# Own term of the first four attention units on TensorE, with more dummies and the gate product moved

## Chip, core and metric

One core of one Trainium2 chip runs the whole kernel. The metric is device time in microseconds (us). Engines are called as in the profile: PE (TensorE, with PEld for its weight loads), DVE (VectorE), ACT (ScalarE), POOL (GpSimd) and SP (SyncE, which issues most of the DMAs).

## What is computed

Three stages follow each other: a linear attention with decays, a dense MLP with a squared ReLU, and a mixture of 8 experts that picks one expert for each token. Only the first has a part in the change:

```python
def _attn_ref(r, k, v, w, u):          # B, H, S, D = 4, 8, 768, 48
    for t in range(S):
        cur = np.einsum('bhd,bhe->bhde', u[None] * kt, vt)
        y[:, :, t] = np.einsum('bhd,bhde->bhe', rt, state + cur)
        state = wt[:, :, :, None] * state + np.einsum('bhd,bhe->bhde', kt, vt)
```

The term `cur` is the token's own term: for head h and token t it adds v[t] times the number sum over d of r[t,d] u[d] k[t,d]. The kernel computes this number for each token and head, and puts it on the diagonal of the matrix of scores. The MLP is `h = max(x @ w_in, 0); (h * h) @ w_out`, and the gate of the experts is a product with the MLP's output.

## The kernel before

**Tiling.** The 768 tokens fall into C = 6 chunks of T = 128. A *unit* (c, b) is chunk c of batch b, with all 8 heads as PAIRS = 4 pairs; 24 units in all. Features lie on partitions: the first head of a pair on partitions 0 to 47, the second on 64 to 111, and the 16 between are padded. `rk_in` holds r and k in this layout, `w_dec` the decays. The MLP of chunk i runs on PE while the attention of chunk i + 1 goes on at its side. So only the four units of chunk 0 stand alone, ahead of everything; the change touches these.

**One unit.** `decays` (DVE, L1193, a scan) makes running products `cum` of the decays; `inverse` (DVE, L1207, two halves) their reciprocals. On POOL `receptance` (L1604) multiplies r by `cum`, `keys` (L1625) k by the reciprocals. On PE `head_scores` (L654) makes the scores. `own_rows` (POOL, L1614 and L1616) multiplies r, k and u from a second copy of r and k with tokens on partitions (`own`, 384 KB a unit, loaded by `load_own`, L406); `own_term` (DVE, L1227) sums over each head's 48 features into `own_sum`; `own_diagonal` (ACT, L978) writes eight diagonal matrices into `scores`. `mask_scores` (DVE, L1215, two instructions) lays the scores above the diagonal over them; it waits for `ps_scores` and `sb_diag`. Then PE goes on with `k_transpose` (L663), `attention` (L683 to L693) and `growth` (L729). ACT takes `k_nat` (L956) and `xt_hi` (L965, `take_xhi`), DVE `xt_lo` (L1259, `take_xlo`). The last `take_xlo` of chunk 0 releases `layer1` of the MLP (L602 to L604).

**Order.** Each engine has its own program, in an order written by hand, and they meet only in semaphores. For chunk 0 this order stands at L832 to L843 (PE), L1085 to L1100 (ACT), L1453 to L1480 (DVE) and L1699 to L1708 (POOL); SP's list of loads begins at L461. `keep_busy(n)` (L830) issues n dummy products of 128x512 on PE, which nobody reads: six ahead of unit 0, two behind the scores of units 1 and 2. `gate_product(0)` (L740) is an unrelated product for the gate, of `gate_w` with 768 KB of transposed `w_out` (`load_transposed(0)`, L425); it stands behind unit 2's growth. `split_hi` (ACT, L944) and `split_lo` (DVE, L1418, or POOL, L1653) split the MLP's weights (`load_mlp_piece`, L420, 768 KB each) into two parts. `early_decays`, `early_rk` and `early_v` are loads for unit n that wait until unit n - 2 is done with the buffer. SP issues in order, so that a load behind a waiting one waits too.

**Buffers.** `own` lies in `spare`, for the odd units of chunk 0 in `stage[1]`. HID[0] and HID[1] are the two PSUM banks of layer 1, unused ahead of it but for the dummies (HID[1]).

Of the kernel before, what the change touches and what calls it, by code (L numbers as in the profile page):

```python
# [18 lines left out]
ALU = mybir.AluOpType  # L19
# [7 lines left out]
T = 128  # L27
# [6 lines left out]
def build(nc, rkw, rk_rows, v, u_rows, w_in, w_out, w_out_t, w_gate, w1, w2, out):  # L34
# [29 lines left out]
    with ExitStack() as ctx:  # L64
        def sb(name, shape, dt=F32):
            return ctx.enter_context(nc.sbuf_tensor(name, shape, dt))
# [57 lines left out]
        k_nat = sb("k_nat", [T, PAIRS, PK])  # L124

# [79 lines left out]
        u_loaded = sem("u_loaded")  # L205
        pad_set = sem("pad_set")
# [164 lines left out]
        def _(sp):  # L371
# [26 lines left out]
            def load_own(c, b):  # L398

                unit = B * c + b  # L400
                if isinstance(c, int) and 2 <= unit <= B:
                    sp.wait_ge(own_summed, unit - 1)
                elif not isinstance(c, int) or unit > 2:
                    sp.wait_ge(own_summed, unit)
                unit = unit % UNITS
                sp.dma_start(own_of(c, b), rk_rows[bass.ds(unit, 1)].rearrange("x t d -> (x t) d")  # L406
                             ).then_inc(own_loaded[b % 2], 16)
# [56 lines left out]
            load_own(0, 0)  # L464
            sp.dma_start(own_u[:, :], u_rows).then_inc(u_loaded, 16)
            load_rk(0, 0, 1)
            sp.wait_ge(const_v, 2)
            load_rk(0, 0, 0)
            load_decays(0, 1, 1)
# [4 lines left out]
            load_own(0, 1)  # L474
# [4 lines left out]
            load_own(0, 2)  # L479
# [4 lines left out]
            load_own(0, 3)  # L484
            load_transposed(0)
            early_rk(3)
            early_v(3)
            early_decays(4)
            load_own(1, 0)
            load_mlp_piece(1)  # L490
# [108 lines left out]
        def _(pe):  # L599
# [232 lines left out]
            keep_busy(6)  # L832
            for b in range(B):
                head_scores(0, b)
                if b == 1 or b == 2:
                    keep_busy(2)
                k_transpose(0, b)
                attention(0, b)
                growth(0, b)
                if b == 2:  # L840
                    pe.wait_ge(const_dma, 16)
                    gate_product(0)
# [97 lines left out]
        def _(act):  # L940
# [40 lines left out]

            def side(n, c, cg, par, c_last, per=8):
# [102 lines left out]
            keep_decay(0)  # L1085
            own_diagonal(0, 0)
            keep_decay(1)
            for b in range(B):
                if b == 1:
                    split_hi(0)  # L1090
                if b == 1 or b == 2:
                    keep_decay(b + 1)
                if b == 3:
                    take_gate(0)
                    split_hi(1)
                take_k(0, b)
                if b < B - 1:
                    own_diagonal(0, b + 1)
                take_xhi(0, 0, b)
# [81 lines left out]
        def _(dve):  # L1181
# [38 lines left out]
            def own_term(c, b):  # L1220

                unit = B * c + b
                n = b % 2
                dve.wait_ge(own_done, 2 * unit + 2)
                if not isinstance(c, int) or unit > 1:
                    dve.wait_ge(sb_diag, unit - 1)
                dve.tensor_reduce(own_sum[:, n, :], own_of(c, b)[:, 0:DM].rearrange("p (h d) -> p h d", h=H), AX.X,  # L1227
                                  ALU.add).then_inc(own_summed, 1)
# [209 lines left out]
            dve.memset(x_cur[:, 0:KD * GW], 0.0)  # L1438
            dve.memset(rk_in[0][32:64].rearrange("p a j t -> p (a j t)"), 1.0).then_inc(const_v, 1)
# [15 lines left out]
            own_term(0, 0)  # L1455
# [5 lines left out]
            own_term(0, 1)  # L1461
            for b in range(2):
                decays(0, b + 2)
                inverses(0, b + 2)
                mask_scores(0, b + 1, 0)
                mask_scores(0, b + 1, 1)
                own_term(0, b + 2)
                take_xlo(0, 0, b)
# [4 lines left out]
            own_term(1, 0)  # L1473
            take_xlo(0, 0, 2)
            take_xlo(0, 0, 3)
            inverse(1, 0, 0)
# [114 lines left out]
        def _(pool):  # L1591
# [14 lines left out]
            def own_rows(c, b):  # L1606

                unit = B * c + b
                n = b % 2
                pool.wait_ge(own_loaded[n], (2 * c + b // 2) * 16 + 16)  # L1610
                if isinstance(c, int) and unit == 0:
                    pool.wait_ge(u_loaded, 16)
                rows = own_of(c, b)
                pool.tensor_tensor(rows[:, 0:DM], rows[:, 0:DM], rows[:, DM:2 * DM], ALU.mult).then_inc(own_done, 1)  # L1614
                pool.wait_ge(own_done, 2 * unit + 1)
                pool.tensor_tensor(rows[:, 0:DM], rows[:, 0:DM], own_u[:, :], ALU.mult).then_inc(own_done, 1)  # L1616

# [10 lines left out]
            def factors(c, b, own_first=False):  # L1628

                if own_first:  # L1630
                    own_rows(c, b)
                    receptance(c, b)
                else:
                    receptance(c, b)
                    own_rows(c, b)
                keys(c, b)
# [62 lines left out]
            for b in range(2):  # L1699
                factors(0, b, own_first=True)  # L1700
            own_rows(0, 2)
            receptance(0, 2)
            keys(0, 2)
            factors(0, 3, own_first=True)
# [112 lines left out]
```

## Time and profile before

| | |
|---|---|
| median of 3 runs | 778.81 us (777.79 to 779.17) |
| the profiled execution | 779.41 us |
| its span | 777.8 us |
| busy: PE, DVE, ACT, POOL | 755.1, 469.6, 323.7, 229.3 us |
| granted clock over the span | 0.991 |
| first product of layer 1 starts at | 40.75 us |

The four units of chunk 0, from the timelines (start of the instruction, us):

| unit | scores (PE) | diagonal (ACT) | mask (DVE) | transposes (PE) | PE idle ahead of them |
|---|---|---|---|---|---|
| (0,0) | 12.48 | 9.76 | 13.82 | 15.21 | 1.56 |
| (0,1) | 18.26 | 17.50 | 22.61 | 23.95 | 2.02 |
| (0,2) | 25.98 | 25.68 | 29.47 | 30.81 | 1.75 |
| (0,3) | 33.64 | 32.55 | 35.20 | 36.58 | 1.78 |

How to read it: a row of a timeline has the start and the length of an instruction, engine, line, operation and tiles (written <- read); brackets show how long the engine had been idle and who released it. Line numbers are those of the kernel before. The chain of waits is followed back from the last instruction, at each step to what released it. PEclk is the granted share of TensorE's full clock: 1.00 is 2.4 GHz, 0.50 is 1.2 GHz.

### The profile page before, as it was taken

The page shows a single profiled execution, that of the slowest core. Times are in us where ns is not written, and L with a number is a line of the kernel's source. Part 1 is how long each engine was busy: PE and PEld are TensorE (multiplying, and loading weights), DVE is VectorE, ACT ScalarE, POOL GpSimd, SP SyncE. Part 2 cuts the span into 40 slices and gives each one's busy share as a digit, 9 for nine tenths or more (in the row PEclk, how much of TensorE's full clock was granted, in tenths as well). Part 3 has the DMA queues.
Part 4 walks back from the last instruction along what each step waited for, and adds up shares of the span by engine and source line. Part 5 has one row for each costly group of instructions (what it writes and reads, how often), then busy time and mean ns, then how long its engine had stood idle before and what let it go on. Part 6 is the DMA issues. An engine that isn't in the chain of part 4 may idle for free.

```text
span 777.8 us, 15695 instructions
## 1 busy us (share of the span) xinstructions
PE 755.1 (97%) x5571; PEld 661.1 (85%) x5571; DVE 469.6 (60%) x756; ACT 323.7 (42%) x636; POOL 229.3 (29%) x213
## 2 busy tenths in 40 slices
PE   6799999999999999999999999999999999999994
PEld 3488888888988888888888899998999999999994
DVE  8977887866586576676486645334542246353861
ACT  3555544434333334434344323253432255253841
POOL 7834423312242222421042210262431112211211
PEclk9999999999999999999999999999999999999998
DMA  9875222321132223322331005154661126616610
GB/s 231 270 227 186 69 67 86 109 62 41 44 111 63 62 63 102 93 62 62 101 95 40 23 33 203 58 190 138 227 233 61 61 62 214 224 55 224 212 52 7
DMA packets 50195, 87.99 MB, mean 113 GB/s; under 512 B 5932, under 2 KB 33560, under 8 KB 50128
## 3 DMA queue, kind: packets, MB, share of 16 engines
q1 hardware_dynamic: 41376, 61.01, 27.5%
q0 software_dynamic: 7648, 24.51, 8.7%
q10 hardware_dynamic: 1104, 1.57, 0.6%
q8 instruction: 43, 0.70, 0.4%
q14 instruction: 24, 0.20, 0.1%
HBM read 72.78 MB, written 16.75 MB: 115 GB/s over the span
## 4 chain that ended last, share of the span: by engine, by line
PE 91%; DVE 3%; ACT 1%; issue 1%; POOL 1%; DMA 1%; SPq 0%; DVEq 0%; POOLq 0%; ACTq 0%
PE bank L602 27%; PE bank L604 25%; PE bank L603 25%; PE bank L654 3%; PE bank L874 3%; PE bank L683 2%; PE bank L699 2%; PE bank L729 1%; PE bank L663 1%; PE bank L821 1%; ACT spare L978 1%; DVE spare L1215 1%; DVE work L1193 1%; PE bank L688 1%; PE bank L693 1%
## 5 line engine op out<-in xcount | busy, mean ns | idle before, releaser
L602 PE MATMUL bank<-wo_hi,h_hi 128*128 128x394 f32 (+1 forms) x576 | 201.6, 350 | 1.0 <-DVE h_lo L1505 1.0
L604 PE MATMUL bank<-wo_hi,h_lo 128*128 128x394 f32 (+1 forms) x576 | 196.1, 340 | 0.0
L603 PE MATMUL bank<-wo_lo,h_hi 128*128 128x394 f32 (+1 forms) x576 | 195.6, 340 | 0.0
L1383 DVE SCALAR_TENSOR_TENSOR hid<-bank,hid 128x512 f32<-128x512 f32 x96 | 65.2, 679 | 135.0 <-ACT hid L1020 135.0
L1020 ACT ACTIVATE hid<-bank 128x512 f32<-128x512 f32 x96 | 57.0, 594 | 158.3 <-PE bank L604 149.9
L602 PE MATMUL bank<-xt_hi,wi_hi 128*128 128x512 f32 x288 | 116.5, 405 | 0.3 <-DVE xt_lo L1259 0.3
L602 PEld LDWEIGHTS bank<-wo_hi,h_hi 128*128 128x128 f32 x576 | 108.3, 188 | 9.0 <-issue 3.0
L604 PE MATMUL bank<-xt_hi,wi_lo 128*128 128x512 f32 x288 | 113.0, 392 | 0.0
L603 PE MATMUL bank<-xt_lo,wi_hi 128*128 128x512 f32 x288 | 112.7, 391 | 0.0
L603 PEld LDWEIGHTS bank<-wo_lo,h_hi 128*128 128x128 f32 x576 | 108.5, 188 | 2.9
L1604 POOL TENSOR_TENSOR work<-work 112x512 f32<-112x512 f32 x24 | 35.6, 1484 | 251.6 <-DVE work L1193 249.7
L604 PEld LDWEIGHTS bank<-wo_hi,h_lo 128*128 128x128 f32 x576 | 108.4, 188 | 0.0
L1029 ACT ACTIVATE h_hi<-hid 128x512 fp32r<-128x512 f32 x96 | 60.6, 631 | 86.3 <-DVE hid L1383 85.2
L1744 POOL DMA_INDIRECT out<-odds,y_idx x26 | 26.9, 1033 | 172.4 <-DVE odds L1517 153.7
L1389 DVE TENSOR_TENSOR h_lo<-hid,h_hi 128x512 fp32r<-128x512 f32 x96 | 66.5, 693 | 17.6 <-ACT h_hi L1029 17.2
L1207 DVE RECIPROCAL odds<-work 112x256 f32<-112x256 f32 x44 | 76.6, 1745 | 0.7
L978 ACT ACTIVATE spare<-ident,own_sum 128x128 f32<-128x128 f32 x192 | 58.7, 388 | 33.4 <-DVE own_sum L1227 27.1
L1111 ACT ACTIVATE hid<-bank 128x512 f32<-128x512 f32 x48 | 28.7, 597 | 87.7 <-PE bank L604 81.7
L604 PEld LDWEIGHTS bank<-xt_hi,wi_lo 128*128 128x128 f32 x288 | 54.0, 188 | 12.3
L602 PEld LDWEIGHTS bank<-xt_hi,wi_hi 128*128 128x128 f32 x288 | 54.0, 188 | 11.9 <-issue 2.0
L1322 DVE TENSOR_TENSOR xt_lo<-bank,xt_hi 128x384 fp32r<-128x384 f32 x25 | 13.9, 557 | 81.8 <-ACT xt_hi L1038 81.8
L603 PEld LDWEIGHTS bank<-xt_lo,wi_hi 128*128 128x128 f32 x288 | 54.1, 188 | 8.3
(152 smaller groups left out, 1221.3 us busy)
## 6 DMA issues: line engine op xcount, KB each, us to landing
work<-rkw SPq DMA_DIRECT2D x48, 192.0 KB, 3.8
spare<-rk_rows SPq DMA_DIRECT2D x22, 384.0 KB, 4.2
work<-sorted_rows SPq DMA_DIRECT2D x24, 193.0 KB
work<-rkw SPq DMA_DIRECT2D x48, 96.0 KB, 3.3
work<-v_rows SPq DMA_DIRECT2D x24, 192.0 KB, 3.9
x_cur<-sorted_rows SPq DMA_DIRECT2D x24, 192.0 KB
work<-w POOLq DMA_DIRECT2D x6, 768.0 KB, 7.4
x<-w POOLq DMA_DIRECT2D x6, 768.0 KB, 10.1
```

The source lines that it names most:

```text
L602: pe.matmul(ps, a_hi, b_hi, start=start, stop=False, skip_group_check=True)
L603: pe.matmul(ps, a_hi, b_lo, start=False, stop=False, skip_group_check=True)
L604: return pe.matmul(ps, a_lo, b_hi, start=False, stop=stop, skip_group_check=True)
L978: last = act.activation(scores[:, h % 2, h // 2, :], ident[:, :], ACT.Copy, scale=own_sum[:, b % 2, h:h + 1])
L1020: act.activation(hid[:, f % 2, :], HID[f % 2][:, :], ACT.Relu).then_inc(sb_relu, 1)
L1029: act.activation(h_hi[:, f % 3, :], hid[:, f % 2, :], ACT.Copy).then_inc(sb_hhi, 1)
L1111: act.activation(hid[:, half, :], banks[2 + half][:, :], ACT.Relu).then_inc(e_relu, 1)
L1207: dve.reciprocal(inv_of(c, b)[0:PK, :].rearrange("p (j t) -> p j t", j=PAIRS)[:, two], by_time(cum[b % 2])[0:PK, two, 1:T + 1]).then_inc(i ...
L1383: dve.scalar_tensor_tensor(hid[:, f % 2, :], HID[f % 2][:, :], 0.0, hid[:, f % 2, :], ALU.max, ALU.mult).then_inc(sb_sq, 1)
L1389: dve.tensor_tensor(h_lo[:, f % 3, :], hid[:, f % 2, :], h_hi[:, f % 3, :].bitcast(F32), ALU.subtract).then_inc(sb_hlo, 1)
L1604: pool.tensor_tensor(r, r, by_time(cum[n])[0:PK, :, 0:T], ALU.mult).then_inc(r_done, 1)
L1744: pool.indirect_dma_start(out=out, out_offset=bass.IndirectOffsetOnAxis(ap=y_idx[:, n:n + 1], axis=0), in_=y_out[:, n, :], in_offset=None, ...
```

## The change

The own term of units (0,0) to (0,3) is made in another way; from unit (1,0) on it is as before.

- POOL: `first_own(b)` multiplies r by k in the layout with features on partitions, ahead of `receptance`, one instruction of 112x512 in place of the two of `own_rows`. It needs the unit's `rk` load only.
- PE: `own_products(b)` multiplies this product (as the stationary side, 112x128 a pair) by `u_two`, four products with two columns, which sums over the features and weights by u. It writes 8 columns of HID[0]. For unit 0 it stands between three and two dummies, for units 1 to 3 behind the attention of the unit before and ahead of its growth.
- ACT: `take_own(b)` copies 128x8 from PSUM to `own_sum`, ahead of the diagonal. DVE's `own_term` is gone for these units, and that of (1,0) stands behind the last two `take_xlo`.
- SP: the loads of `own` for these units are gone; `u_two` comes in two small loads of single elements; `own_u` and `own (1,0)` come later; `load_mlp_piece(1)` comes earlier, `load_transposed(0)` later, behind the loads of unit 3 and ahead of `early_decays(4)`.
- Dummies: 3 + 2 ahead of unit 0 (6 before), one behind the scores of unit 0 (none), two for units 1 and 2 as before, one for unit 3 (none). `gate_product(0)` moves from behind unit 2's growth to behind unit 3's scores. ACT's `split_hi(1)` moves from unit 3 to unit 2.

```diff
@@ SP
-            load_own(0, 0)
-            sp.dma_start(own_u[:, :], u_rows).then_inc(u_loaded, 16)
             load_rk(0, 0, 1)
             sp.wait_ge(const_v, 2)
             load_rk(0, 0, 0)
+            for half in range(2):
+                p = slice(HALF * half, HALF * half + D)
+                src = u_rows[0:1, :].rearrange("x (j a d) -> a d (x j)", a=2, d=D)
+                sp.dma_start(u_two[p, :, half], src[half], allow_slow_non_contiguous=True).then_inc(u_two_loaded, 16)
...
-            load_own(0, 1)
...
-            load_own(0, 2)
             load_mlp_piece(0)
             early_decays(3)
             early_rk(2)
             early_v(2)
-            load_own(0, 3)
-            load_transposed(0)
+            load_mlp_piece(1)
             early_rk(3)
             early_v(3)
+            load_transposed(0)
             early_decays(4)
+            sp.dma_start(own_u[:, :], u_rows).then_inc(u_loaded, 16)
             load_own(1, 0)
-            load_mlp_piece(1)
@@ PE
+            def own_products(b):
+                pe.wait_ge(own_done, 2 * b + 2)
+                if b > 0:
+                    pe.wait_ge(own_summed, b)
+                rows = by_time(own_of(0, b)[:, 0:PAIRS * T])
+                for j in range(PAIRS):
+                    last = pe.matmul(HID[0][:, 2 * j:2 * j + 2], rows[0:PK, j, :], u_two[0:PK, j, :],
+                                     start=(j == 0), stop=(j == PAIRS - 1), skip_group_check=True)
+                last.then_inc(ps_own, 1)
-            keep_busy(6)
+            keep_busy(3)
+            pe.wait_ge(u_two_loaded, 32)
+            own_products(0)
+            keep_busy(2)
             for b in range(B):
                 head_scores(0, b)
-                if b == 1 or b == 2:
+                if b == 0:
+                    keep_busy(1)
+                elif b < B - 1:
                     keep_busy(2)
+                else:
+                    pe.wait_ge(const_dma, 16)
+                    gate_product(0)
+                    keep_busy(1)
                 k_transpose(0, b)
                 attention(0, b)
+                if b < B - 1:
+                    own_products(b + 1)
                 growth(0, b)
-                if b == 2:
-                    pe.wait_ge(const_dma, 16)
-                    gate_product(0)
@@ ACT
+            def take_own(b):
+                act.wait_ge(ps_own, b + 1)
+                act.activation(own_sum[:, b % 2, :], HID[0][:, 0:H], ACT.Copy).then_inc(own_summed, 1)
             keep_decay(0)
+            take_own(0)
             own_diagonal(0, 0)
...
+                if b == 2:
+                    split_hi(1)
                 if b == 3:
                     take_gate(0)
-                    split_hi(1)
                 take_k(0, b)
                 if b < B - 1:
+                    take_own(b + 1)
                     own_diagonal(0, b + 1)
                 take_xhi(0, 0, b)
@@ DVE
+            dve.memset(u_two[:, :, :], 0.0)
...
-            own_term(0, 0)
...
-            own_term(0, 1)
...
-                own_term(0, b + 2)
...
-            own_term(1, 0)
             take_xlo(0, 0, 2)
             take_xlo(0, 0, 3)
+            own_term(1, 0)
@@ POOL
+            def first_own(b):
+                pool.wait_ge(loaded[b % 2], (b // 2) * 32 + 32)
+                if b > 1:
+                    pool.wait_ge(own_summed, b - 1)
+                pool.tensor_tensor(by_time(own_of(0, b)[:, 0:PAIRS * T])[0:PK], rk_in[b % 2][0:PK, 0],
+                                   rk_in[b % 2][0:PK, 1], ALU.mult).then_inc(own_done, 2)
-            for b in range(2):
-                factors(0, b, own_first=True)
-            own_rows(0, 2)
-            receptance(0, 2)
-            keys(0, 2)
-            factors(0, 3, own_first=True)
+            for b in range(B):
+                first_own(b)
+                receptance(0, b)
+                keys(0, b)
```

## Rows read from the trace of the kernel before

**Rows 1.** Stretches of the trace: busy us of each engine (instructions), granted clock, DMA share.

```profile
40.75:777.00 736.25, 726.38 (x5254) 643.04 (x5254) 434.75 (x715) 305.22 (x587) 195.34 (x173) 1.00 0.34 105
```

**Rows 2.** The chain of waits, 0 to 50 us: start, us, what ended last.

```profile
39.52 0.50 ACT xt_hi L965
40.05 0.57 DVE xt_lo L1259
```

**Rows 3.** DVE's timeline, 4 to 36 us: start, us, engine, line, operation, tiles.

```profile
5.50 3.36 DVE L1207 RECIPROCAL odds<-work 112x256 f32<-112x256 f32 x2
...
13.82 1.34 DVE L1215 COPY_PREDICATED spare<-before,bank 128x512 f32<-128x512 int32 x2 [0.66 <-PE bank L654]
...
16.70 0.50 DVE L1227 TENSOR_REDUCE own_sum<-stage 128x8 f32<-128x384 f32 x1
17.11 2.18 DVE L1193 TENSOR_TENSOR_SCAN work<-work,odds 112x516 f32<-112x516 f32 x1
...
22.61 1.28 DVE L1215 COPY_PREDICATED spare<-before,bank 128x512 f32<-128x512 int32 x2
...
24.70 1.46 DVE L1193 TENSOR_TENSOR_SCAN work<-work,odds 112x516 f32<-112x516 f32 x1
...
29.47 1.28 DVE L1215 COPY_PREDICATED spare<-before,bank 128x512 f32<-128x512 int32 x2
...
33.54 1.73 DVE L1418 TENSOR_TENSOR wi_lo<-stage,wi_hi 128x1536 fp32r<-128x1536 f32 x1
35.20 1.33 DVE L1215 COPY_PREDICATED spare<-before,bank 128x512 f32<-128x512 int32 x2
```

**Rows 4.** ACT's timeline, 30 to 41 us, the diagonal and a small copy.

```profile
32.55 2.45 ACT L978 ACTIVATE spare<-ident,own_sum 128x128 f32<-128x128 f32 x8 [0.56 <-PE bank L683]
...
40.50 0.20 ACT L1077 ACTIVATE wo_hi<-bank 128x40 fp32r<-128x40 f32 x1 [0.49 <-PE bank L748]
```

**Rows 5.** Stretches again: the granted clock (column PEclk) behind two pauses of PE.

```profile
16.00:20.00 4.00, 3.94 (x65) 3.26 (x55) 3.96 (x4) 2.89 (x10) 3.07 (x2) 0.57 1.08 274
36.60:40.00 3.40, 3.40 (x52) 2.63 (x52) 0.82 (x2) 1.33 (x3) 3.40 (x5) 0.50 1.01 370
```

**Rows 6.** POOL's timeline: one receptance, keys (0,0), keys (0,1).

```profile
9.10 1.18 POOL L1604 TENSOR_TENSOR work<-work 112x512 f32<-112x512 f32 x1
10.23 2.20 POOL L1625 TENSOR_TENSOR work<-work,odds 112x512 f32<-112x512 f32 x1
...
16.93 1.27 POOL L1625 TENSOR_TENSOR work<-work,hid 112x512 f32<-112x512 f32 x1 [0.99 <-DVE hid L1207]
```

**Rows 7.** PE's weight loads of the dummies, 8 to 10 us.

```profile
8.55 0.34 PEld L830 LDWEIGHTS bank<-odds,before 128*128 128x128 f32 x1 [0.52 <-issue]
9.35 0.19 PEld L830 LDWEIGHTS bank<-odds,before 128*128 128x128 f32 x1 [0.46 <-issue]
```

**Rows 8.** PE's timeline, 12 to 31 us: scores, two dummies, transposes.

```profile
12.48 1.16 PE L654 MATMUL bank<-work 48*128 48x128 f32 x16 [0.40 <-POOL work L1625]
...
19.94 1.98 PE L830 MATMUL bank<-odds,before 128*128 128x512 f32 x4
...
30.81 0.60 PE L663 MATMUL bank<-ident,work 112*128 112x112 f32 x4 [1.75 <-DVE spare L1215]
```

**Rows 9.** DMA issues, 24.5 to 27.4 us: line, KB each, us to landing.

```profile
work<-rkw SPq DMA_DIRECT2D x2, 192.0 KB, 3.2
```

**Rows 10.** DMA issues, 19.0 to 19.5 us.

```profile
x<-w_out_t SPq DMA_DIRECT2D x1, 768.0 KB, 6.4
```

**Rows 11.** DMA issues, 6.4 to 7.1 us.

```profile
work<-v_rows SPq DMA_DIRECT2D x1, 192.0 KB, 7.2
x_cur<-w_gate SPq DMA_DIRECT2D x1, 15.0 KB, 7.0
```

**Rows 12.** DMA issues, 35.2 to 36.5 us.

```profile
stage<-w_out SPq DMA_DIRECT2D x1, 768.0 KB, 10.1
work<-rkw SPq DMA_DIRECT2D x2, 96.0 KB, 8.8
```

More of the change, by code:

```diff
@@ L124, in build @@
         k_nat = sb("k_nat", [T, PAIRS, PK])
+        u_two = sb("u_two", [T, PAIRS, 2])
         state = spare[:, 2 * DM + 8 * T:].rearrange("p (b j d) -> p b j d", b=B, j=PAIRS)
@@ L205, in build @@
         u_loaded = sem("u_loaded")
+        u_two_loaded = sem("u_two_loaded")
+        ps_own = sem("ps_own")
         pad_set = sem("pad_set")
@@ L400, in load_own @@
                 unit = B * c + b
[L401 to L404, printed above, removed]
+                sp.wait_ge(own_summed, B - 1 if isinstance(c, int) and unit == B else unit)
                 unit = unit % UNITS
@@ L1224, in own_term @@
                 dve.wait_ge(own_done, 2 * unit + 2)
-                if not isinstance(c, int) or unit > 1:
-                    dve.wait_ge(sb_diag, unit - 1)
+                dve.wait_ge(sb_diag, unit - 1)
                 dve.tensor_reduce(own_sum[:, n, :], own_of(c, b)[:, 0:DM].rearrange("p (h d) -> p h d", h=H), AX.X,
@@ L1609, in own_rows @@
                 n = b % 2
-                pool.wait_ge(own_loaded[n], (2 * c + b // 2) * 16 + 16)
-                if isinstance(c, int) and unit == 0:
+                pool.wait_ge(own_loaded[n], (2 * c + b // 2 - 2) * 16 + 16)
+                if isinstance(c, int) and unit == B:
                     pool.wait_ge(u_loaded, 16)
@@ L1626, in keys, with factors @@
                                    ).then_inc(k_done, 1)
[L1628 to L1635, printed above, removed]
+            def factors(c, b):
+                receptance(c, b)
+                own_rows(c, b)
                 keys(c, b)
```

## The prediction

> **What bounds the kernel now.** I read first the busy time by stretch [rows 1]. From 40.75 us on, where chunk 0 of the first layer begins, PE is busy in 726.4 of the 736.25 us that are left. Nothing of the change touches these products, so the change can pay only by letting that first layer start earlier, and what it shifts there is carried to the end one for one.
>
> Then the chain of waits of the stretch ahead [rows 2]. It enters through the load of `own_u` and POOL's own rows of unit 0, and ends with attention (0,3), `take_xhi` at 39.52 and `take_xlo` at 40.05. Between them it runs mostly through DVE, whose timeline [rows 3] the reader should lay out as a row of masks: (0,0) at 13.82, (0,1) at 22.61, (0,2) at 29.47, (0,3) at 35.20, each 1.3 us. From 13.82 to 36.5 DVE has no pause. So the units are paced by DVE, except where the diagonal on ACT is later. For unit 3 it is nearly so: ACT's diagonal runs 32.55 to 35.00 [rows 4], DVE's `split_lo(0)` 33.54 to 35.27, and the mask starts at 35.20.
>
> Last, the clock. From 36.6 to 40 PE is granted 0.50, the 1.2 GHz level [rows 5], after it had had nothing to do between the scores and the transposes of unit 3. Unit 3 takes 39.52 - 36.53 = 2.99 us from the end of its mask to the end of attention; unit 2, at 2.4 GHz, 32.55 - 30.75 = 1.80.
>
> **Part by part, first the start.** Removed from POOL: two products in each of units 0 to 3, and four loads of 384 KB. Added: one product of r and k of the shape of `receptance`, 1.18 us [rows 6]. `own_u` leaves the first queue places. The first product needs `rk(0,0)` alone, which now has two decay halves ahead of it; I put its landing at 6.1 us. The product ends at about 7.3, receptance at 8.5, and keys wait for the reciprocals, which end at 8.86 as now [rows 3]. DVE goes straight on to the scan of unit 1, and keys then share their time with it as at 10.23, where they took 2.20 us [rows 6]: 9.0 to 11.3, not 12.43.
>
> This gain of 1.1 us is not all kept, since PE's own queue is now in the way. Passes of a dummy come 0.85 us apart until 9.2 and 0.43 after that; the weight loads show the step from 0.34 to 0.19 us [rows 7]. Three dummies are six passes, 4.15 to 9.25. Then come the four own products, eight passes with two columns each. No row shows such a product. Bounds: a pass of the scores costs 1.16/16 = 0.07 us, one of the transposes, which also load wide weights, 0.60/4 = 0.15 [rows 8]; so 0.6 to 1.2 us. I take 0.85, between them. Two more dummies are 4 passes, 1.72 us by the row of four in 1.98, less the tail. Scores (0,0): 9.25 + 0.85 + 1.72 = 11.8, to 13.0; the mask starts at 13.15 after 13.82, a gain of 0.7. The diagonal is ready just before: products out at 10.2, `take_own` 0.20 like the small copy of [rows 4], diagonal 2.45, so 13.0.
>
> The Trainium skill, "TensorE: Matmul & The Clock Gate", section "LDWEIGHTS (loading the stationary operand)", has the load's time as columns/1.2, however little streams after it: it speaks against using 128 weight columns for 2 results. An estimate by it is 8 x 107 ns = 0.86 us, and the sum would come out the same.
>
> **DVE from mask to mask.** After mask (0,0), one reciprocal of 1.75 us ends at 16.1. Before, `own_term` (16.70 to 17.1) followed, and then the scan took 2.18 us because keys (0,1) had started 0.18 us ahead of it [rows 3, 6]. Now the scan comes directly, ahead of POOL, and takes 1.23: it ends at 17.4, not 19.3. Two reciprocals of 3.4: mask (0,1) at 20.75, gain 1.85. POOL's keys (0,1) end at 18.7, scores at 19.9: not late. The next scan, 24.70 now, would be due at 22.4, but rk(0,2) is issued at 15.2, lands 3.2 to 4 us after its issue where little is queued [rows 9], and then product, receptance and keys follow, 1.2 each: keys hold the port until about 23.2 and the scan ends at 24.4. Mask (0,2) at 27.7, gain 1.8.
>
> **Unit 3, where the added wait sits.** Removed: `own_term` from DVE. Added, in series: own products on PE behind attention (0,2), 0.85, then `take_own`, 0.20, and two hand-overs, 0.1. The diagonal waited for attention alone until now, and the last mask is queued behind it. From the end of mask (0,2), 29.0: attention ends at 30.7 (+1.7 as in unit 2), diagonal starts at 31.85, ends at 34.3, mask at 34.45. So 1.8 shrinks to 0.75 us. For units 1 and 2 the same wait is covered: their diagonals end at 19.8 and 27.4, ahead of masks at 20.75 and 27.7.
>
> Other waits into this mask: the scan of (1,0) needs `early_decays(4)`, now behind the 768 KB of `load_transposed(0)`, which itself moved from 19.12 to about 24.9. The queue then holds some 1.3 MB at about 300 KB/us, so the decays land at 30.6; scan 1.25 and split 1.73 [rows 3] end at 33.6, 0.8 us before they cost anything.
>
> **The clock and the gate product.** Between scores and transposes of unit 3 PE now has the gate product (0.86 us) and a dummy (0.86), and its pause shrinks to under 1 us. If it keeps 2.4 GHz, this returns 2.99 - 1.80 = 1.2 us. Cost of the gate product: it needs `transposed`, issued at 24.9; by the 6.4 us of [rows 10] it lands at 31.3 at the latest, scores (0,3) end at 32.8. It is hidden, with the two ending at 34.5, a us before the transposes can start.
>
> **Costed at nothing:** the two `u_two` loads, 384 elements of 4 B. The gate weights came as 384 pieces of 40 B and landed 0.27 us after the v rows ahead of them (6.92 + 7.0 against 6.45 + 7.2) [rows 11]; `u_two` has until 9.25. The Trainium skill, "DMA: Bandwidth & Descriptors", section "Rules for kernel authors", warns that such a load becomes one descriptor for each element; the trace's 0.27 us for as many pieces decides. `own_term(1,0)` moves behind the last `take_xlo` and delays the first `square` by 0.5 us; layer 1 has its other bank, so PE does not see it. Dummies of units 0 and 1 lie in pauses that masks end.
>
> **The sum.** Mask (0,3) 0.75 us earlier, 1.2 us of clock: 1.95, call it 2.0. The profiled execution has 779.41 us (span 777.8, 1.6 around it), 0.6 over the median of 778.81. By its own sum it becomes 777.4, and the median 776.8 us. A measurement can tell about 0.2%, 1.56 us, from no change.
>
> **Rivals.** (1) The clock is 1.2 GHz in unit 3 all the same: the pause is shorter but there, and between 16 and 20 us, behind the pause ahead of 15.2, PE also had 0.57 [rows 5]. Then 0.8 us of gain stays: 778.0. Against it: units 1 and 2 have two dummies in this place, and their transposes run at 2.4 (0.60 us, as the row of unit 2 has it [rows 8]).
> (2) The diagonal's new wait is longer (own products at their upper bound or at 1.2 GHz, up to +0.85), so that the last mask is no earlier than now: 777.6 to 778.
> (3) Slower: `early_decays(4)` behind the transposed weights. The same load issued at 35.7 behind three large pieces took 8.8 us, and the last of these pieces 10.1 [rows 12]. Issued at 25.5 the decays would land at 34.3 to 35.6, the last mask would start at 37.4 to 38.7, 2.2 to 3.5 us later than before, and the clock gives 1.2 back: 779.8 to 781.1. It costs from a landing of 31.4 on and turns the whole change into a loss from 33.4. Against it: fewer bytes are queued than at 35.7.
> (4) It does not do what it says: POOL and DVE are relieved, but scans and keys fall into each other's time otherwise than I laid out (a scan held as the one of 2.18 us), 0.9 us lost at one of three places: 777.8.
> (5) More than forecast: own products at 0.07 us a pass, keys (0,2) earlier: 776.0.
>
> **How the numbers follow.** Forecast 776.8, 0.50; (5) 0.08; (1) 0.15; (2) and (4) together 0.17; (3) 0.10. Faster by over 0.2% (under 777.25): 0.58, the forecast and (5); slower (over 780.4): 0.07, the upper part of (3); within it 0.35, the rest. Range 775.6 to 779.1: the lower end is (5) with 0.4 for the spread of the runs, the upper end takes in (1) and (4) with that spread and leaves out most of (3).
>
> **What would show it.** Masks of DVE at 13.1, 20.8, 27.7 and 34.4; an own product of about 0.85 us after each attention; diagonal (0,3) starting 1.1 us after attention (0,2) ended; a granted clock of 1.00 at the transposes of unit 3; the first product of layer 1 at 38.8. A pause of DVE ahead of the scan of (1,0) would be rival 3, a long wait of the gate product the same load seen from PE. The forecast is wrong if the stretch after 40 us isn't carried one for one.

## The result and the profile after

| | before | after |
|---|---|---|
| median, us (12 runs each) | 778.74 (777.79 to 779.25) | 783.23 (779.96 to 784.25) |
| the profiled execution, its span, us | 779.41, 777.8 | 783.07, 781.5 |
| granted clock over the span | 0.991 | 0.991 |
| first product of layer 1 at, us | 40.75 | 40.30 |

The ratio of after to before is 1.0053, interval 1.0043 to 1.0064: the change makes the kernel slower by half a per cent, where 776.8 us was forecast and 775.6 to 779.1 was the range.

The stretch that the change touches is not where it went. Layer 1 starts 0.45 us earlier than before. The lead can be followed through DVE's copies of `logits`, one mark for each chunk: 298.76 against 299.19 us in before, still 0.43 ahead, and then 388.53 against 384.00, 4.53 behind.

DVE's timeline of before and of after around 300 us, start, us, engine, line, operation, tiles, and in brackets the idle time ahead and its releaser; before is the first fence.

```profile
299.19 0.24 DVE L1395 COPY logits<-bank 128x10 f32<-128x10 f32 x2 [2.53 <-PE bank L604]
299.36 1.02 DVE L1404 COPY x<-bank 128x384 f32<-128x384 f32 x2
301.94 0.69 DVE L1383 SCALAR_TENSOR_TENSOR hid<-bank,hid 128x512 f32<-128x512 f32 x1 [1.56 <-ACT hid L1020]
302.55 1.37 DVE L1215 COPY_PREDICATED spare<-before,bank 128x512 f32<-128x512 int32 x2
...
304.40 1.23 DVE L1193 TENSOR_TENSOR_SCAN work<-work,odds 112x516 f32<-112x516 f32 x1
...
384.00 0.24 DVE L1395 COPY logits<-bank 128x10 f32<-128x10 f32 x2 [2.53 <-PE bank L604]
```

```profile
298.76 0.24 DVE L1422 COPY logits<-bank 128x10 f32<-128x10 f32 x2 [2.53 <-PE bank L604]
298.93 1.02 DVE L1431 COPY x<-bank 128x384 f32<-128x384 f32 x2
303.36 0.69 DVE L1410 SCALAR_TENSOR_TENSOR hid<-bank,hid 128x512 f32<-128x512 f32 x1 [3.41 <-issue]
306.02 1.33 DVE L1243 COPY_PREDICATED spare<-before,bank 128x512 f32<-128x512 int32 x2 [1.97 <-issue]
...
307.84 1.22 DVE L1221 TENSOR_TENSOR_SCAN work<-work,odds 112x516 f32<-112x516 f32 x1
...
388.53 0.24 DVE L1422 COPY logits<-bank 128x10 f32<-128x10 f32 x2 [2.53 <-PE bank L604]
```

In before DVE's pause at 300.4 ends with ACT's `hid`, which it needed. In after ACT's `hid` is done at 300.92 + 0.60 = 301.52, and DVE starts at 303.36, released by "issue", which is time in which it waited for nothing that the profile shows; behind this one instruction comes a second such pause. The scan is at 307.84 against 304.40: the 0.43 us of lead have become 3.44 of lag. Two things mark the place. It is where DVE's loop over two chunks at a time (L1510 of after, `dve.Fori`) jumps back to its start, for the only time (it runs twice). And the DMA view shows loads of instructions there. Its rows for 299 to 308 us (queue, kind, packets, MB, share of 16 engines), first before, then after:

```profile
q8 instruction: 1, 0.02, 0.6%
```

```profile
q14 instruction: 3, 0.02, 0.8%
```

The row of q8 doesn't belong to the jump: between 200 and 480 us a load of 16 KB on q8 comes about every 10 to 25 us in both traces, in after at 308.7, just behind the window. The three of 8 KB on q14 are what is new. By the trace they start at 301.3, 304.0 and 306.5 us, behind the jump, while before has no load on q14 between 282.7 and 313.1.

The chain of waits of after, 295 to 312 us (start, us, what ended last), runs through the pause, and PE's own rows (stretch: length, busy of PE, PEld, DVE, ACT and POOL, granted clock, DMA share, GB/s) show who pays, before first:

```profile
299.06 0.07 DVEq L1510
299.13 0.28 issue
299.41 0.55 DVE x L1431
299.95 3.27 issue
303.22 0.09 DVEq L1510
303.36 0.10 DVE hid L1410
303.46 2.35 issue
```

```profile
299.95:306.20 6.25, 6.25 (x83) 5.09 (x85) 4.66 (x7) 2.65 (x6) 0.49 (x1) 1.00 0.65 213
```

```profile
299.95:306.20 6.25, 4.21 (x29) 2.96 (x27) 0.88 (x3) 1.71 (x3) 0.00 (x0) 1.00 0.59 203
...
304.00:308.00 4.00, 0.76 (x4) 0.60 (x4) 2.03 (x5) 1.11 (x2) 0.00 (x0) 0.91 0.01 4
308.00:312.00 4.00, 4.00 (x63) 3.16 (x62) 3.96 (x4) 1.04 (x2) 2.78 (x3) 0.66 0.02 4
```

PE runs dry behind DVE (0.76 us busy of the 4 from 304 on), and as it comes back the granted clock falls: 0.66 from 308 to 312, where before had 1.00. That is where the further 1.1 us from +3.44 to +4.53 go. On PE itself the transposes of this unit come 3.00 us later than in before (the two rows below, before first), and from them to the next product of layer 1 PE takes 3.73 us (307.40 to 311.13) where before took 2.15 (304.40 to 306.55), for the same work: 3.00 + 1.58 = 4.58 behind. At the end of the span +3.7 is left.

```profile
304.40 0.55 PE L663 MATMUL bank<-ident,work 112*128 112x112 f32 x4
```

```profile
307.40 1.01 PE L663 MATMUL bank<-ident,work 112*128 112x112 f32 x4 [3.24 <-DVE spare L1243]
```

**The stretch ahead of layer 1.** Rows of after that answer to [rows 3, 4, 5, 8], from the timelines of DVE, PE and ACT and the view of stretches:

```profile
13.89 1.33 DVE L1243 COPY_PREDICATED spare<-before,bank 128x512 f32<-128x512 int32 x2 [1.96 <-PE bank L654]
...
21.26 1.30 DVE L1243 COPY_PREDICATED spare<-before,bank 128x512 f32<-128x512 int32 x2
...
29.02 1.36 DVE L1243 COPY_PREDICATED spare<-before,bank 128x512 f32<-128x512 int32 x2 [0.75 <-ACT spare L998]
33.20 1.23 DVE L1221 TENSOR_TENSOR_SCAN work<-work,odds 112x516 f32<-112x516 f32 x1 [2.38 <-DMA work<-rkw]
34.35 1.73 DVE L1445 TENSOR_TENSOR wi_lo<-stage,wi_hi 128x1536 fp32r<-128x1536 f32 x1
36.00 1.34 DVE L1243 COPY_PREDICATED spare<-before,bank 128x512 f32<-128x512 int32 x2
```

```profile
9.41 1.40 PE L840 MATMUL bank<-u_two,spare 112*128 112x2 f32 x8
...
20.15 3.40 PE L830 MATMUL bank<-odds,before 128*128 128x512 f32 x4
23.34 0.86 PE L663 MATMUL bank<-ident,work 112*128 112x112 f32 x4
```

```profile
33.28 2.45 ACT L998 ACTIVATE spare<-ident,own_sum 128x128 f32<-128x128 f32 x8
```

```profile
22.00:24.00 2.00, 2.00 (x6) 0.78 (x4) 2.00 (x3) 0.41 (x2) 1.78 (x2) 0.50 0.89 334
36.60:40.00 3.40, 2.37 (x53) 1.79 (x53) 1.57 (x4) 1.24 (x3) 3.32 (x4) 1.00 1.03 379
```

The clock came back in unit 3 as forecast (1.00 where [rows 5] have 0.50). But it fell in unit 1: the same four passes of dummies that took 1.98 us in [rows 8] took 3.40, and the transposes behind them came 0.78 us after the mask's end (22.56). Unit 2's mask then waited 0.75 us for its diagonal. And the scan of unit (1,0) waited 2.38 us for its decays; through it and the split the last mask was at 36.00, 0.80 later than in before.

### The profile page after: what moved, and what is told of

Read it like the earlier page. It is cut to its first block, busy times and chain, and to the rows that moved or that the text cites. A ratio compares the mean times of both kernels' runs of the same rounds, so it can differ in the third digit from the quotient of the medians.

```text
span 781.5 us, 15764 instructions
## 1 busy us (share of the span) xinstructions
PE 760.3 (97%) x5605; PEld 664.9 (85%) x5605; DVE 467.6 (60%) x753; ACT 324.5 (42%) x640; POOL 223.0 (29%) x209
## 4 chain that ended last, share of the span: by engine, by line
PE 92%; DVE 3%; issue 2%; DMA 1%; ACT 1%; SPq 0%; DVEq 0%; POOL 0%; POOLq 0%; ACTq 0%
PE bank L602 27%; PE bank L604 25%; PE bank L603 25%; PE bank L654 3%; PE bank L894 3%; PE bank L699 2%; PE bank L683 2%; PE bank L830 1%; PE bank L729 1%; PE bank L663 1%; PE bank L821 1%; DMA work<-rkw 1%; PE bank L688 1%; PE bank L693 1%; DVE spare L1243 1%
```

## Experiments

Theory A: DVE's loss at 300 us is a wait for its own instructions at the loop's jump back, and whether there is one hangs on where the loop lies in DVE's program. Ahead of the jump's branch DVE's trace has 531 instructions of all kinds in before and 526 in after (four `own_term` and two waits less, one memset more). Theory B: it is a consequence of the change's work or timing, such as later loads, the clock, or POOL and DVE meeting otherwise.

**The five instructions put back, as ones that do nothing** (one column each of a tile that nobody reads).

```diff
@@ DVE, before the first decays
+            for n in range(5):
+                dve.memset(unused[:, n:n + 1], 0.0)
```

> The changed kernel, with five one-column memsets of a tile that nobody reads, on DVE ahead of mask (0,0), where DVE waits anyway. The change takes five instructions (four own terms and two waits gone, one memset new) from DVE's program ahead of its loop over chunks; in its trace DVE stands still for 3.41 and 1.97 us at 300 us, where the loop's first pass ends, with three 8 KB instruction loads beside it. Theory (the loop's place in DVE's program decides whether its code has to be loaded again at the jump): the pauses at 300 us go, the span falls by 3.5 to 4.2 us to about 777.3, the time is about 779.0. Rival (the pause comes from PE's or ACT's longer program, or from the data loads): it stays, 783.2 as before the pads. Rival (the time went into the clock drop at 21 us): 783.2 too, with the pause gone but something else late.

Measured: 778.24 us (776.78 to 779.64), 0.9982 of before [0.9971, 0.9992]. The pauses are gone, and so are the three loads on q14; the DMA view of the stretch has only the usual one on q8:

```profile
q8 instruction: 1, 0.02, 0.6%
```

So 5.0 us of the medians' difference (783.23 - 778.24) go with five instructions that compute nothing, 5.5 by the ratios. In this profile, which is that of the slowest of its ten runs (779.64), layer 1 starts at 40.95, 0.20 later than in before, since the clock fell in unit 1 and the decays were waited for (a scan at 33.85 behind a wait of 3.62 us), and the span is 778.0, 0.2 over before's: here the shift is carried one for one.

**The kernel before with three DVE instructions fewer**, nothing of the change in it.

```diff
@@ DVE, before the first decays (bounds and y_idx: to behind the loop)
-            dve.memset(bounds[:, 0:2], 0)
-            dve.memset(y_idx[:, :], int(FAR))
-            dve.memset(ones_b[:, :], 1.0)
@@ POOL
+            pool.memset(ones_b[:, :], 1.0)
```

> The kernel before, with three DVE instructions fewer ahead of the loop (two memsets put behind it, the memset of ones_b given to POOL) and nothing else. Theory of the loop's place: if the edge lies within three instructions, the same pauses at 300 us appear and the time rises by some 4 us, to 782.8; if the edge lies at the fourth or fifth, nothing happens (778.7). Rival (the pauses need the own products, the new loads or PE's new program): 778.7 whatever the edge. So a rise proves the theory, no rise leaves it open.

Measured: 786.4 us (786.1 to 787.06), 1.0095 [1.0077, 1.0113]. Three instructions fewer cost the old kernel 7.4 us by the ratio, and the pause is in the same place, again with three loads on q14:

```profile
306.36 0.69 DVE L1383 SCALAR_TENSOR_TENSOR hid<-bank,hid 128x512 f32<-128x512 f32 x1 [6.23 <-issue]
```

Up to 299 us this profile is 0.25 ahead of before, from 350 us on 6.6 behind. This rules B out for the pause: no own product, no moved load is in it.

**Where the edge lies.** The five memsets as two, and as four.

```diff
-            for n in range(5):
+            for n in range(2):        # and range(4)
```

> The changed kernel with two memsets on DVE in place of five, so that its loop lies three instructions nearer to the start of the program than in the kernel before. Theory of the loop's place: as in the kernel before with three fewer, DVE stands still at 300 us, 3 us or more in all, and the time is 781.5 to 786. Rival (the pads helped in another way, such as by moving the first mask): no pause, 778.2.

> The same with four memsets, one short of the place that the loop has in the kernel before. It finds the edge: a pause at 300 us says that the edge lies within the last instruction, none that it lies at the second or third. Both are open to the theory; a time near 778.2 without the pause, 781.5 or more with it.

Measured: two give 781.57 us (780.09 to 782.34), 1.0029 [1.0013, 1.0044]; four give 777.67 (776.19 to 778.63), 0.9977 [0.9961, 0.9993]. With two, layer 1 starts 2.70 us ahead of before, keeps that until 299, and lies 3.6 behind at the next mark (387.64). The first row is of the kernel with two, the second of that with four, which has no pause:

```profile
303.61 0.69 DVE L1411 SCALAR_TENSOR_TENSOR hid<-bank,hid 128x512 f32<-128x512 f32 x1 [5.93 <-issue]
```

```profile
299.63 0.69 DVE L1411 SCALAR_TENSOR_TENSOR hid<-bank,hid 128x512 f32<-128x512 f32 x1 [1.60 <-ACT hid L1046]
```

Counted to the jump's branch, 526 and 528 instructions pause (528 in two kernels: after with two, before less three), 530 and 531 don't.

**Is it the length of the program or the loop's place in it?** Five memsets behind the loop.

```diff
@@ DVE, behind the loop over chunks
+            for n in range(5):
+                dve.memset(unused[:, n:n + 1], 0.0)
```

> The changed kernel with the five unused memsets on DVE behind its loop over chunks instead of ahead of it. Theory of the loop's place: the loop lies where the changed kernel has it, so DVE stands still at 300 us as there, 4 to 6 us in all, time 781.5 to 784. Rival (the longer program or the memsets as such help): no pause, about 778.

Measured: 783.86 us (783.2 to 785.8), 1.0058 [1.0034, 1.0083]. The program is as long as with five ahead, and has the same two pauses as after. So it is the place of the loop and not the length.

```profile
303.87 0.69 DVE L1411 SCALAR_TENSOR_TENSOR hid<-bank,hid 128x512 f32<-128x512 f32 x1 [3.75 <-issue]
306.52 1.33 DVE L1244 COPY_PREDICATED spare<-before,bank 128x512 f32<-128x512 int32 x2 [1.96 <-issue]
```

**The clock's part alone:** the kernel before with `gate_product(0)` and one dummy at unit 3's scores.

```diff
@@ PE
+                if b == 3:
+                    pe.wait_ge(const_dma, 16)
+                    gate_product(0)
+                    keep_busy(1)
                 k_transpose(0, b)
                 attention(0, b)
                 growth(0, b)
-                if b == 2:
-                    pe.wait_ge(const_dma, 16)
-                    gate_product(0)
```

> The kernel before with one part of the change alone: gate product and one dummy behind unit 3's scores, nothing else. DVE's program is untouched. Theory (this part returns unit 3's time at 1.2 GHz): end of mask (0,3) to the end of attention falls from 2.99 to 1.8 us, the time to 777.5. Rival (clock drops all the same, or the two products end after the mask, at 34.8 + 1.7 = 36.5): no gain, 778.7.

Measured: 779.18 us (778.39 to 780.63), 1.0002 [0.9992, 1.0013]. The mechanism is in the profile: the clock is 1.00 from 36.6 to 38.6, the mask's end at 36.63 to `xt_hi` at 38.36 takes 1.73 us, against 2.99 and the 1.80 that I took for 2.4 GHz, and layer 1 starts at 39.59, 1.16 earlier. The medians don't show it. Its span, 777.0, is 0.8 under before's. But this profile is not typical of its kernel: its granted clock over the span is 0.994, which one more of the ten runs has, and the other eight have 0.990 (0.991 in the profile of before). So in most runs more of the span was at the lower clock, and where that lay no trace shows.

**The other two delays of unit 3's mask, with the five memsets in.** First only the order of loads; then only the order on PE (own products ahead of the transposes, `take_own` ahead of `take_k`); then both, which was in fact run first.

```diff
@@ SP (loads)                          @@ PE (order)
+            early_decays(4)           +                if b < B - 1:
             load_transposed(0)        +                    own_products(b + 1)
-            early_decays(4)                            k_transpose(0, b)
                                                        attention(0, b)
                                       -                if b < B - 1:
                                       -                    own_products(b + 1)
```

> The changed kernel with five pads and early_decays(4) behind early_v(2), own products where the change has them. Theory 1 (the load behind the transposed weights cost what DVE waited for it, 2.38 us in the changed kernel's trace): the scan of (1,0) starts at about 31 and mask (0,3) 0.3 us earlier, bounded by the diagonal; 777.9. Theory 2, after the run with both edits (keys (0,3) took 3.91 us beside scan and split there, and the mask waited 2.5 us for the scores): scan and split now hold POOL's keys (0,3) up, mask (0,3) no earlier or later; 778.5 to 780. Then DVE's wait for the load was no loss but room for POOL.

> The changed kernel with five pads and each own product ahead of the unit's transposes, loads as in the changed kernel. Theory (the diagonal's new wait is what took the gain of mask (0,3)): diagonal (0,3) starts right behind attention (0,2), as before the change, 1.2 us earlier, but the mask still waits for scan and split behind their load, so the time stays within 0.5 us of the pads alone, 778.2. Rival (own products and dummies, now in one pause, end after the mask): transposes of units 1 and 2 start 0.5 to 2 us later than the mask allows, time 779 to 780.

> The changed kernel with the five pads, with early_decays(4) issued behind early_v(2) instead of behind load_transposed(0), and with each own product ahead of the unit's transposes (in PE's pause) instead of behind its attention, take_own ahead of take_k. In the changed kernel's trace two things end together ahead of mask (0,3) at 36.00: split_lo(0), late by the 2.38 us for which the scan of (1,0) waited for its load (landed 33.2), and the diagonal, which ended at 35.7 because own products and take_own stood between attention and it. Theory (both together hold the last mask): it starts 1.2 to 2 us earlier, and the time is 777.0 to 777.8, that is 1.2 to 2 below the pads alone. Rival (DVE and POOL pace it anyway): equal to the pads alone, 779.0.

Measured: loads 777.35 us (776.16 to 778.08), 0.9976 [0.9965, 0.9987]; order 776.07 (775.75 to 777.19), 0.9969 [0.9955, 0.9983]; both 780.81 (778.7 to 781.34), 1.0011 [1.0001, 1.0021]. Against the five memsets alone (0.9982) either is no loss, and both together are one; the loads came near the 777.9 of their theory, the order on PE gained where none was expected, and both together missed the 777.0 to 777.8 of theirs. With the loads alone the scan comes at 29.74 and the mask is left waiting for the diagonal. With the order alone the diagonal starts at 30.30, and the mask waits behind scan and split. DVE's rows, first loads, then order:

```profile
34.88 1.34 DVE L1244 COPY_PREDICATED spare<-before,bank 128x512 f32<-128x512 int32 x2 [1.32 <-ACT spare L999]
```

```profile
31.60 1.23 DVE L1223 TENSOR_TENSOR_SCAN work<-work,odds 112x516 f32<-112x516 f32 x1 [2.82 <-DMA work<-rkw]
...
34.40 1.34 DVE L1245 COPY_PREDICATED spare<-before,bank 128x512 f32<-128x512 int32 x2
```

With both, DVE's scan (30.02, 2.09 us) and split (32.03, 1.73 us) lie beside POOL's keys of unit 3, and the scores wait 2.00 us for the keys. The rows of POOL, then of DVE:

```profile
30.98 3.91 POOL L1662 TENSOR_TENSOR work<-work,hid 112x512 f32<-112x512 f32 x1
```

```profile
36.27 1.36 DVE L1245 COPY_PREDICATED spare<-before,bank 128x512 f32<-128x512 int32 x2 [2.52 <-PE bank L655]
```

An instruction of this shape took 1.27 us alone and 2.20 beside one scan [rows 6]. PE also fell to 0.50 twice in this profile, in units 1 and 3, and layer 1 started at 42.23. The wait for the keys is rival (4) of the prediction, made by hand. But it is the smaller part of the loss. Layer 1 starts 3.53 us later than with the order alone: 1.25 of this is there at mask (0,2), 28.31 against 27.06, ahead of these keys; 0.62 comes from there to the last mask; and 1.66 behind that mask, where the clock was at 0.50. Whether the longer wait of PE brought that fall is not shown.

**Split behind the mask.** The loads' order again, with `split_lo(0)` moved behind the last mask; then that with the order on PE, and one dummy fewer in unit 1.

```diff
@@ DVE                                 @@ PE (the second kernel only)
             decays(1, 0)                                 elif b < B - 1:
-            split_lo(0)               -                    keep_busy(2)
             mask_scores(0, 3, 0)      +                    keep_busy(b)
             mask_scores(0, 3, 1)
             take_xlo(0, 0, 2)
+            split_lo(0)
```

> The changed kernel with five pads, early_decays(4) behind early_v(2), and DVE's split_lo(0) behind the mask and take_xlo of unit (0,3) instead of ahead of them; own products behind the attention. Theory (diagonal wait and split both stood ahead of the last mask): the mask is now bound by the diagonal alone, as with the earlier load only, where it started at 34.88 after 1.32 us of waiting for the diagonal; so no more gain than there, 777.3. Rival (keys of unit 3 were held up by the split): the scores come earlier, but the mask does not, the same 777.3; a time under 776.5 would speak against the diagonal as the last wait.

> As the last, and each own product ahead of the unit's transposes, and one dummy instead of two behind the scores of unit 1. Theory (with own products early the diagonal starts right behind the attention, and with load and split out of the way nothing else holds the last mask): mask (0,3) starts about 1.5 us earlier than with the early own products alone (34.40 there), first product of layer 1 at 37.2, time 774.6 to 775.3. Rival (keys (0,3) beside the scan, or a clock drop behind the longer pauses of PE, take it back): 776 or more, with transposes or scores of unit 3 at 1.2 GHz.

Measured: 778.32 us (776.62 to 779.79), 0.9982 [0.9971, 0.9994], and 777.2 (775.63 to 781.38), 0.9973 [0.9957, 0.9988]. In both the last mask waits for the diagonal alone (2.82 and 3.04 us), so the diagonal is the next thing late once load and split are away. The second starts layer 1 at 37.15, the earliest of all and as its theory had it, but the time of 774.6 to 775.3 was missed: the profile is of its best run, 775.63, and its twelve runs spread over 5.7 us, seven with a granted clock of 0.996 or 0.997 (775.6 to 776.5) and five with 0.992 or less (777.9 to 781.4). Neither kernel beats the order on PE alone.

**The best version once more**, the same kernel as "order".

> The changed kernel with five pads and early own products once more, in more rounds, because five runs gave 776.07 us and the version with three further edits 777.2 (775.6 to 781.4). If the early own products as such are worth something over the pads alone (0.9982 and 0.9977 of the kernel before with five and four pads), the ratio is 0.9965 to 0.9975; if the 776.07 was luck in where the clock drops fell, 0.998 or more.

Measured: 775.94 us (775.46 to 775.99), 0.9956 of before [0.9943, 0.9970]. It is faster than both kernels: 0.3 to 0.4% under before in its two sets of runs, and some 7 us under after. Its profile has no fall of the clock ahead of layer 1 or at the jump: span 774.3, granted clock 0.997, layer 1 at 37.71.

What the order on PE is worth seems to lie in the clock rather than in the diagonal. Nine of its ten runs have a granted clock of 0.996 or 0.997. With four or five memsets and the old order only six of 18 have 0.995 or more; of the others, at 0.993 and 0.994, none is under 777.5 us. In the two profiles of the one kernel layer 1 starts at 38.70 and 37.71, against 38.41 with four memsets, so the earlier diagonal shows no gain there. The difference of 1.0 us between the two profiles is that of their last masks (34.40 and 33.41), behind scans of (1,0) that waited for their decays until 31.60 and 30.59. That fewer falls come because an own product now stands in PE's pause is likely, but no run tests it by itself.

## Why the prediction was wrong

**The step that failed** is in the first paragraph: "Nothing of the change touches these products", so "what it shifts there is carried to the end one for one". The change removes five instructions from DVE's program ahead of a loop that runs 250 us later. I priced the instructions that go (as time of DVE) and not the place of those that stay. The stop there cost 3.87 us (from -0.43 to +3.44), and another 1.1 goes with the fall of the clock behind it. Where there is no stop, the sentence holds to within half a us: -2.34 at layer 1 and -2.8 at the end with four memsets, +0.20 and +0.2 with five, +1.48 and +1.6 with both orders changed. The last paragraph did name this as what would make the forecast wrong, but no rival was made of it, and so it had no price.

The Trainium skill, "Runtime: NRT & Kernel Launch", section "Instruction fetch mechanics", has an engine hold two pages of its program and fetch ahead only in sequence; a taken branch to a page outside must wait for the fetch. The stops fit that rule, with the loads on q14 beside each; that q14 is DVE's own queue is inferred from this, and no view names it. The rule alone would not have told which kernel stops: at the same jump four of the kernels shown stop (3.41 and 1.97, 3.75 and 1.96, 5.93, 6.23 us), and before doesn't.

**Ahead of layer 1, step by step.** The kernel with four memsets is after without the stop, and its profile had no fall of the clock, so it is the one that the sum was made for. It is a lucky run of its kernel: 776.62 us, with a median of 777.67. Its rows of DVE, PE and ACT:

```profile
12.63 1.34 DVE L1244 COPY_PREDICATED spare<-before,bank 128x512 f32<-128x512 int32 x2 [0.64 <-PE bank L655]
...
20.00 1.29 DVE L1244 COPY_PREDICATED spare<-before,bank 128x512 f32<-128x512 int32 x2
...
26.77 1.35 DVE L1244 COPY_PREDICATED spare<-before,bank 128x512 f32<-128x512 int32 x2
31.31 1.23 DVE L1222 TENSOR_TENSOR_SCAN work<-work,odds 112x516 f32<-112x516 f32 x1 [2.75 <-DMA work<-rkw]
...
34.11 1.33 DVE L1244 COPY_PREDICATED spare<-before,bank 128x512 f32<-128x512 int32 x2
```

```profile
8.34 0.95 PE L841 MATMUL bank<-u_two,spare 112*128 112x2 f32 x8
...
29.72 1.05 PE L841 MATMUL bank<-u_two,stage 112*128 112x2 f32 x8
```

```profile
31.02 2.45 ACT L999 ACTIVATE spare<-ident,own_sum 128x128 f32<-128x128 f32 x8
```

| step | forecast | four memsets | after |
|---|---|---|---|
| mask (0,0) | 13.15 | 12.63 | 13.89 |
| mask (0,1) | 20.75 | 20.00 | 21.26 |
| mask (0,2) | 27.7 | 26.77 | 29.02 |
| mask (0,3) | 34.45 | 34.11 | 36.00 |
| own products, us | 0.85 | 0.95 to 1.05 | 1.05, the first 1.40 |
| diagonal (0,3) | 31.85 | 31.02 | 33.28 |
| scan (1,0) | not late | 31.31, late | 33.20, late |
| first product of layer 1 | 38.8 | 38.41 | 40.30 |

- Own products: inside the bounds of 0.6 to 1.2, above the value taken. The first of after took 1.40: PE was still slow there, since a weight load of it at 8.56 us took 0.34 us, as those of the first dummies do, where later ones take 0.19 [rows 7]. The column of the granted clock doesn't show this; it has 1.00 from 9 to 11.
- The diagonal's new wait, from the end of mask (0,2) to the diagonal of unit 3: 28.12 to 31.02 = 2.90 us, 1.10 over before's 1.80; forecast 1.15. So the size of this wait is right to 0.05. That it is covered in unit 2 held with four memsets, but not in after, where the mask waited 0.75 us for the diagonal.
- The clock in unit 3: right. Mask's end to `xt_hi` takes 1.73 us in after, 2.99 before, so rival (1), which had 1.2 GHz there all the same, did not come true. What I had not priced is a fall in unit 1. "Dummies of units 0 and 1 lie in pauses that masks end" fails with it: at a granted 0.50 the four passes of unit 1 outlast the mask. After lies 1.89 us behind the four-memset kernel at layer 1: 1.26 from unit 0, whose weight loads of the dummies come down from 0.34 to 0.19 us later (the one at 7.48 us has 0.19 with four memsets), 0.99 from unit 1 with its fall (mask (0,1) to mask (0,2) takes 7.76 against 6.77), and 0.36 of this came back in unit 3.
- Rival (3) was half there. The decays were forecast at 30.6, 0.8 before they cost anything. They came at 31.31 and 33.20, and in both kernels the scan and split behind them, not the diagonal, released the last mask (diagonals end at 33.47 and 35.73, masks start 34.11 and 36.00). The price was at most 0.64 and 0.27 us, not the 2.2 to 3.5 of the rival. This landing moves much from profile to profile: with the loads as the change has them, the scan that waits for it starts between 30.59 and 33.85 us.
- Costed at nothing, and right but for the dummies: the small loads of `u_two` (the own product of unit 0 follows the dummies with no wait in after), the gate product (34.55 to 35.41, ahead of the mask), the later `own_term(1,0)` (PE waits 0.54 us for `xt_lo` at 40.30 and then runs on).

So the sum for the start was good in its terms, with some luck in the total. Without the stop the kernel takes 777.67 us with four memsets and 778.24 with five, a gain of 1.8 and 1.4 us by the ratios for a forecast of 2.0. In the four-memset profile unit 0 came half a us before the forecast since PE sped up before the 9.25 us that the sum took from before; from there to layer 1 it took 25.78 us, for a forecast of 25.65. The sum came 6.4 us under the measured 783.23. By the profiles, 783.07 less 777.4 is 5.7: 1.5 at layer 1 (unit 0's slow start and the fall in unit 1), 4.96 from there to 388 us (the stop and the fall behind it), less 0.8 that comes back after 388.

## What to carry to other kernels

An edit ahead of a loop moves the loop's code in the program of the engine that it takes instructions from or gives them to. The runs show this for DVE alone; for the other engines it is worth a look. Before trusting that a gain is carried to the end, follow the difference between two traces by one repeated mark, and look at each loop's jump back for "issue" pauses and instruction loads. A few instructions that do nothing, added or taken away ahead of the loop, tell in one run whether an edit is being judged by its work or by its place.

## What the runs showed of the hardware

- A loop's jump back stops DVE for up to 6.2 us or not at all. With 526 and 528 instructions in DVE's trace ahead of the jump's branch it stops, with 530 and 531 it doesn't; each stop comes with three loads of 8 KB of instructions on q14, where the others have none. Why the edge is there is not shown, nor whether further edges come.
- The clock's falls to 0.50 lie in other places from profile to profile: before has two (one ahead of 20 us, one in unit 3), after one in unit 1 and one behind the stop, the kernel with four memsets and the best version none of these. They also differ among the runs of one kernel: after has a granted clock of 0.990 to 0.996 and 784.25 to 779.96 us, and with four memsets three of eight runs have 0.996 (776.2 to 776.6 us) and five 0.994 (777.6 to 778.6). So one profile doesn't tell where a kernel's clock falls. The runs show no rule that would have told it.
- Eight passes with 128 weight columns and two columns of data took 0.95 to 1.05 us at a granted clock of 1.00 once PE had sped up, 0.12 to 0.13 a pass, close to the 0.15 of a transpose's pass [rows 8], though they stream two columns where it streams 112.
